# A looped part that is never entered, a lookup table handed over in two parts, and one transfer for q, k and the decay logits

## What is computed

```python
f = 1.0 / (1.0 + np.exp(-f_logit))
for t in range(S):
    state = f[:, :, t, :, None] * state + np.einsum('bhd,bhe->bhde', k[:, :, t], v[:, :, t])
    y[:, :, t] = np.einsum('bhd,bhde->bhe', q[:, :, t], state)
x = attn_out.transpose(0, 2, 1, 3).reshape(B * S, H * D)

logits = x @ w_gate + modality_bias[modality_id]
e_idx = np.argmax(logits, axis=1)
probs = np.exp(logits - logits.max(-1, keepdims=True)); probs /= probs.sum(-1, keepdims=True) + 1e-09
h = np.maximum(x[mask] @ w1[e], 0.0)
out[mask] = gate_w[mask, None] * (h @ w2[e])          # for each expert e

g = xn @ w_gate                                        # xn: x after RMS norm
return ((g * (1.0 / (1.0 + np.exp(-g)))) * (xn @ w_val)) @ w_out
```

## Time and profile before

| | us |
|---|---|
| median of 3 executions | 838.8 (836.85 to 844.91) |
| the profiled execution, its own time | 838.23 |
| its span, first to last instruction | 836.5 |
| TensorE busy in the span | 811.1 (97%) |
| DVE, ACT, GpSimd busy | 452.0, 380.0, 140.5 |

### The profile page before, as it was taken

How to read it: one execution, slowest core, us unless ns; L and a number is a source line. 1 busy time by engine, 2 the same in 40 slices (tenths; PEclk the granted TensorE clock), 3 DMA queues, 4 the chain that set the end, 5 groups by cost and what they waited for, 6 DMA issues and landing times.

```text
span 836.5 us, 15683 instructions
## 1 busy us (share of the span) xinstructions
PE 811.1 (97%) x5624; PEld 737.0 (88%) x5624; DVE 452.0 (54%) x715; ACT 380.0 (45%) x742; POOL 140.5 (17%) x170
## 2 busy tenths in 40 slices
PE   7999987799999999989999999999999999999997
PEld 6888877799999999988888888888988888888886
DVE  8989996886666666634433433333333334333331
ACT  6999975666665555534223312412332233122222
POOL 4003043785540000000001000200110010001001
PEclk9999998999999999999999999999999999999999
DMA  9979866998887977602002000200100000001000
GB/s 202 198 154 225 174 210 229 339 348 292 255 260 253 355 233 260 174 20 96 1 0 76 1 1 1 75 0 0 51 25 0 0 38 0 0 0 38 0 0 38
DMA packets 44121, 96.59 MB, mean 115 GB/s; under 512 B 9200, under 2 KB 25072, under 8 KB 43952
## 3 DMA queue, kind: packets, MB, share of 16 engines
q1 hardware_dynamic: 39984, 85.81, 34.7%
q0 software_dynamic: 3840, 9.47, 3.2%
q10 hardware_dynamic: 256, 0.79, 0.4%
HBM read 76.75 MB, written 19.29 MB: 115 GB/s over the span
## 4 chain that ended last, share of the span: by engine, by line
PE 88%; DVE 4%; issue 2%; ACT 2%; DMA 1%; POOL 0%; SPq 0%; DVEq 0%; ACTq 0%
PE h_ps L1887 16%; PE h_ps L1888 16%; PE h_ps L1886 16%; PE ym_ps L1886 7%; PE ym_ps L1888 7%; PE ym_ps L1887 7%; PE xTm_ps L1886 3%; PE xTm_ps L1888 3%; PE xTm_ps L1887 3%; PE sc_ps L839 2%; PE x_ps L859 2%; PE yT_ps L811 2%; PE ds_ps L783 1%; PE yT_ps L804 1%; PE turn_ps L830 1%
## 5 line engine op out<-in xcount | busy, mean ns | idle before, releaser
L1862 DVE TENSOR_TENSOR gs<-h_ps,sig 128x512 f32<-128x512 f32 x72 | 49.8, 692 | 177.2 <-ACT sig L1679 177.2
L1679 ACT ACTIVATE sig<-h_ps 128x512 f32<-128x512 f32 x72 | 43.1, 598 | 160.3 <-PE h_ps L1888 160.3
L1690 ACT CAST h_hi<-hid 128x512 fp32r<-128x512 f32 x72 | 44.6, 620 | 149.5 <-DVE hid L1865 149.5
L1886 PE MATMUL h_ps<-x_hi,w_hi 128*128 128x256 f32 x312 | 90.0, 289 | 8.4 <-DVE w_lo L271 4.5
L1887 PE MATMUL h_ps<-x_hi,w_lo 128*128 128x256 f32 x312 | 89.6, 287 | 0.0
L1888 PE MATMUL h_ps<-x_lo,w_hi 128*128 128x256 f32 x312 | 89.6, 287 | 0.0
L1888 PE MATMUL h_ps<-w_lo,wg_hi 128*128 128x512 f32 x216 | 85.2, 395 | 0.0
L1887 PE MATMUL h_ps<-w_hi,wg_lo 128*128 128x512 f32 x216 | 85.1, 394 | 0.0
L1886 PE MATMUL h_ps<-w_hi,wg_hi 128*128 128x512 f32 x216 | 84.1, 389 | 0.0
L1888 PE MATMUL h_ps<-w_lo,wv_hi 128*128 128x512 f32 x216 | 84.1, 389 | 0.0
L1886 PE MATMUL h_ps<-w_hi,wv_hi 128*128 128x512 f32 x216 | 84.0, 389 | 0.0
(11 more groups left out here) (237 smaller groups left out, 1790.3 us busy)
## 6 DMA issues: line engine op xcount, KB each, us to landing
w_raw<-in_w SPq DMA_DIRECT2D x52, 384.0 KB, 5.3
w_in<-in_w SPq DMA_DIRECT2D x52, 384.0 KB, 5.5
qkf_in<-in_qkf SPq DMA_DIRECT2D x43, 288.0 KB, 5.0
y_sorted<-x_tiles SPq DMA_DIRECT2D x13, 384.0 KB, 3.6
v_in<-in_v SPq DMA_DIRECT2D x24, 192.0 KB, 5.3
x_regions<-zero_row SPq DMA_DIRECT2D x12, 384.0 KB, 3.1
x_tiles<-x_regions SPq DMA_DIRECT2D x12, 384.0 KB, 4.0
g_in<-in_wg SPq DMA_DIRECT2D x3, 768.0 KB, 6.9
```

The lines of the kernel that those rows point to most:

```text
L1679: nc.scalar.activation(sig[:], g_ps, ACT.Sigmoid).then_inc(sig_done, 1)
L1690: nc.scalar.copy(h2_hi[:, fb % HELD], hid[:]).then_inc(h2_hi_done, 1)
L1862: nc.vector.tensor_tensor(gs[:], g_ps, sig[:], ALU.mult).then_inc(gs_done, 1)
L1886: nc.tensor.matmul(out, hi, rhs_hi, start=first, stop=False)
```

## The change

1. q, k and f of a tile lie in memory as 112 rows of 6144 bytes, with the 16 neutral rows among them, and one DMA of 112 partitions replaces two of 48 (`FIRST_LOADS` gives the new counts to wait for). The very first loads keep their form.
2. GpSimd no longer waits at the end of attention for its own scatters to land. `least` and `small`, from which the flag comes, are made one pipeline step earlier, and the flag's product stands ahead of `read` on TensorE.
3. In `general_attention` TensorE's part over tiles is a true loop of one body instead of code written out for four tiles and again for the last group. It reads its rows from a buffer `rows_in` of its own.
4. The table is made in two parts. Expert numbers and region ends are written straight to `table` (`table_ready` 1); rows, offsets and the count of tiles follow after `shifted_scores` (`table_ready` 2). SyncE loads w1 part 0 of tile 1 after the first, ahead of `pad`, and x and the later parts after the second.
5. In the first tile `place` stands ahead of `lo_w2(0, 0)`, the tiles of the experts behind lo_h(0), and `rows_of_tiles` and `gates_of_tokens` at the end of the tile instead of inside it. TensorE counts after hidden(0) instead of inside it.
6. ACT spreads its four `hi_w2(0, g)` over the tile, without a wait for SyncE's mark, and does one third of the dense weights (`hi_third(1)`) at the end. In all tiles the parts 2 and 3 of w2 are split at the start of the tile that uses them, not at the end of the one before. GpSimd's thirds wait for `w2_split` at 6 instead of `x_split` at 2.

The core of the diff:

```diff
             def load_qkf(c, b, n):
                 wait_past(sp, scaled, n - 3)
-                for par in range(2):
-                    sp.dma_start(qkf_in[par * PAD:par * PAD + D, b].rearrange("p a j t -> p (a j t)"),
-                                 qkf[n, par]).then_inc(qkf_landed[b], 16)
+                sp.dma_start(qkf_in[0:ROWS, b].rearrange("p a j t -> p (a j t)"), qkf[n]).then_inc(qkf_landed[b], 16)
...
-            for b in range(B):
-                pool.wait_ge(scattered[b], 16 * (LATE // B))
-            pool.wait_ge(scattered_late, 16 * B)
-            pool.wait_ge(ended, 16 * B)
...
-                def group(c):
-                    for b in range(B):
+                with pe.Fori(0, CH) as c:
+                    with pe.Fori(0, B) as b:
...
                 if place == "first":
                     sp.wait_ge(table_ready, 1)
                     e1 = expert(1)
-                    pad(e1)
                     for g in range(GR):
+                        sp.wait_ge(w1_split, g + 1)
+                        load_w1(e1, g)
+                        if g == 0:
+                            pad(e1)
                         if g == 1:
+                            sp.wait_ge(table_ready, 2)
                             sp.wait_ge(scattered, 16 * B)
                             load_x(1)
-                        sp.wait_ge(w1_split, g + 1)
-                        load_w1(e1, g)
...
-            pool.wait_ge(x_split, 2)
+            pool.wait_ge(w2_split, GR + 2)
...
-            lo_w2(0, 0)
             dve.wait_ge(counted, 1)
             rt.place(nc, dve, CH - 1, B, (CH - 1) * B, pre_ps, cnt_ps, marks, 0)
+            lo_w2(0, 0)
...
+                lo_h(0)
                 if place == "first":
                     tiles_of_experts()
-                lo_h(0)
-                if place == "first":
-                    table_of_tiles()
                 else:
+                    lo_w2(j, 2)
                     next_w1(0)
                 lo_h(1)
                 if place == "first":
                     lo_w2(0, 1)
                     shifted_scores()
-                    lo_w2(0, 2)
+                    table_of_tiles()
+                else:
+                    lo_w2(j, 3)
```

More of the change, by code:

```diff
@@ L438, in first_load @@
                 eng.wait_ge(pads_set[b], 1)
[L439 removed]
+                eng.dma_start(qkf_in[rows, b, 2].rearrange("p j t -> p (j t)"), qkf[b, rows, f_cols:]).then_inc(f_landed[b], 16)
             else:
@@ L846, in step @@
                     nc.tensor.matmul(flag_ps, rt.ones_r[:], small[:], start=True, stop=True).then_inc(flag_sum, 1)
+                    read(c, b, tile(c, b, 2))
                     pe.wait_ge(ks_done, GROWN)
@@ L1144, in group @@
                         mm.then_inc(lgt_done, 1)
-                    if not is_last(c):
+                    with pe.If(c < CH - 1):
                         pe.wait_ge(redone, c * Routing.PLACED + Routing.CHOSEN)
                         rt.count(nc, B, group_ps[:, 0], group_ps[:, 1]).then_inc(recounted, 1)
-                groups(pe, group)
                 first.turn(nc, pe, xT_ps, ident, again)
@@ L1607, in scalar @@
             act.wait_ge(shared.ahead.w2_landed, 16 * GR)
-            for g in range(GR):
-                hi_w2(0, g)
+            hi_w2(0, 0)
             def body(j, place):
@@ L1621, in next_w2, with own_w2 @@
                     if place != "last":
-                        act.wait_ge(y_part, j * PARTS + (g + 1 if g < GR - 1 else PARTS))
+                        act.wait_ge(y_part, j * PARTS + g + 1)
                         hi_w2(j + 1, g)
+                def own_w2(g):
+                    if place != "first":
+                        act.wait_ge(y_part, j * PARTS)
+                    hi_w2(j, g)
                 if place == "last":
@@ L1628, in body @@
                 hi_h(0)
-                if place != "first":
+                if place == "first":
+                    hi_w2(0, 1)
+                else:
+                    own_w2(2)
                     next_w1(0)
@@ L1632, in body @@
                 if place == "first":
-                    for i in range(EARLY):
-                        hi_third(i)
+                    own_w2(2)
+                    own_w2(3)
+                    hi_third(0)
                 else:
+                    own_w2(3)
                     next_w1(1)
@@ L1665, in body @@
                     nc.scalar.copy(y_kept_rows[:, s], y_ps[:, s, 0:DM]).then_inc(y_kept, 1)
-                next_w2(3)
+                if place == "first":
+                    next_w2(1)
+                    hi_third(1)
                 if place == "middle":
@@ L1830, in body @@
                 if place == "first":
+                    lo_w2(0, 2)
                     lo_w2(0, 3)
-                    rows_of_tiles()
                     next_w1(0)
@@ L1849, in body @@
                     next_w2(0)
+                    rows_of_tiles()
+                    gates_of_tokens()
                     next_w2(1)
-                next_w2(2)
-                next_w2(3)
             tiles(dve, body)
@@ L1911, in hidden @@
                     for i in range(2):
-                        if place == "first" and g == 0 and i == 1:
-                            pe.wait_ge(marks, Routing.CHOSEN)
-                            rt.count(nc, B, pre_ps, cnt_ps).then_inc(counted, 1)
                         cols = slice(i * P, (i + 1) * P)
@@ L1934, in body @@
                 hidden(0)
+                if place == "first":
+                    pe.wait_ge(marks, Routing.CHOSEN)
+                    rt.count(nc, B, pre_ps, cnt_ps).then_inc(counted, 1)
                 hidden(1)
```

59 lines of the change are left out of this document (32 added, 27 removed).

## The result

The changed kernel takes 851.88 us (median of 6 executions, 849.22 to 858.88) against 840.19 for the kernel before (6 executions): 1.0152 times as long, 95% interval 1.0095 to 1.0209. I had said 833, with a range that ended at 839.5. All ratios here leave out executions more than 1.5% above the fastest of their kernel, four in all: one of e7 (2801.15 us), one of e15 and two of the kernel before beside e9 to e11.

A forecast was written before the change was run, and what follows sets the result against it. TensorE, busy for 97% of 836.5 us, was taken to bound the kernel. From 838.23, -3.9 at tile 1's start and -1.5 + 0.3 in it (-5.1) gave 833.1, said as 833; range 829.5 to 839.5.

The forecast's parts named there:

- the sum: Whole kernel: -3.9 us at tile 1's start and -1.5 + 0.3 in it make -5.1.
- behind 177 us all moves up as a whole: Tiles after 177 us: TensorE has no holes there, so the earlier gain was to carry through unchanged.
- The jump: At attention's end: shorter skipped code starts TensorE 4.3 us earlier, and at full clock, which saves some 2.2 us.
- the sign that the prediction names: At attention's end: first h_ps product within 0.5 us of it, and a granted clock of 1.00 from 131 to 141.
- Loads for tile 1: First tile: earlier loads of w1 and x start tile 1 at 154.2 instead of 158.08, 3.9 us won.
- Tile 1: In tile 1: of the 2.70 us wait for h_lo, 1.5 won and 1.2 stay; 0.3 given back.
- so they fit: Past 165 us: three GpSimd operations in a row cost DVE 2.0 us, within h_lo's slack of 3.0.
- Attention: Steady attention: the 98 KB more that a tile moves stay hidden, so no time is won or lost.
- The rivals: Four outcomes: jump costs 4.5 us (0.27), loads sooner (0.08), GpSimd's thirds on h_lo (0.06), DMA-bound attention (0.04).
- Rival 3: Tiles 1 and 2: GpSimd's later thirds delay h_lo; two groups give +5.6 us, 838.7 or 843; chance 0.06.

The follow-up runs named there:

- e7: The kernel before with only one DMA of 112 partitions for q, k and f instead of two of 48; ratio 0.9998 to the kernel before.
- e15: e1 with SyncE's loads of the thirds behind the loads for the next tile; ratio 1.0062 to the kernel before.
- e9: e3 with GpSimd's subtractions and scatters mixed instead of three subtractions in a row; ratio 1.0003 to the kernel before.
- e11: The kernel before with only GpSimd's subtractions and scatters mixed; ratio 0.9975 to the kernel before.
- e2: The kernel before with only the split of w2's parts 2 and 3 moved into the tile that uses them; ratio 1.0157 to the kernel before.
- e5: The kernel before once more, unchanged, for a second profile; no time or ratio is given.
- e1: The changed kernel with w2's parts 2 and 3 split at the end of the tile before; 845.59 us against 846.69 for the kernel before, ratio 0.9999.
- e3: The changed kernel, late split kept, with SyncE's load of x ahead of the loads of w2's parts 2 and 3; ratio 0.9992 to the kernel before.
- e6: The changed kernel once more, unchanged, timed in turns with the kernel before on one chip; ratio 1.0137.
- e8: e1 with two DMAs of 48 partitions for q, k and f; ratio 1.0001 to the kernel before.
- e12: e3 with `rows_of_tiles` and `gates_of_tokens` back inside the first tile; 833.68 us against 839.1 for the kernel before, ratio 0.9936.
- e4: The kernel before with only TensorE's skipped part made a loop; ratio 1.000 to the kernel before.
- e13: e1 with `rows_of_tiles` and `gates_of_tokens` back inside the first tile; ratio 0.9989 to the kernel before.

## Why the prediction was wrong, point by point

- **The step that failed** is one that the sum does not have. Part 6 of the change splits parts 2 and 3 of w2 in the tile that uses them, in all tiles. I followed it through DVE's order in tile 1 only, and wrote that "behind 177 us all moves up as a whole, since TensorE has no holes there". The absence of holes says nothing of the slack. x was asked for 8.6 us ahead of its use, and some 4 of these are landing. The late split took all of the rest (x is asked for 3.9 to 4.0 us ahead in the later tiles, without a wait), and where GpSimd's thirds lengthen DVE's splits it took more, 2.6 us in the tile shown. I did not ask which of SyncE's loads wait for a split that moves, and what stands behind them. Price: 1.0157 by e2 alone, some 13 us; by the twelfth turn_x 8.5 to 11.4 us more than before in the two profiles of the changed kernel.
- **The jump (-4.3 us at the start, and -2.2 for the clock; in the sum only by way of the loads).** Its reading as a cost of the skipped code's length fell with e5, e2, e7 and e11. I took one execution for a property of the kernel. The block from q8 is no proof either: the same trace has one more between 115 and 121 us and one between 136 and 141, where TensorE is busy throughout. So the sign that the prediction names, no hole in the changed kernel, came true by luck. By the rule of the Trainium skill ("Runtime: NRT & Kernel Launch", section "Instruction fetch mechanics") a jump out of the window of two blocks must wait for a fetch. The traces bear that out neither way: the same code waits 4.46 us once and not at all in four other executions.
- **Loads for tile 1 (start at 154.2, -3.9).** Right in size: 22.8 us behind attention's end against 26.9, -4.1 (22.4 to 22.8 in e1, e3, e6, e8). But the working has two errors that cancel: w1 part 2 was issued 16.0 us behind attention's end (150.34), not 14.9, and landed in 3.9 us (ACT takes it at 154.28), not 5.3. Not all of the 4.1 is the new order's, either. With the old order and no hole tile 1 starts at 24.1 (e2) to 26.3 (e7). The rest, 1.3 to 3.9 us, is left to the earlier table with the loads behind it, which no run tried alone.
- **Tile 1 (-1.2).** 2.38 us of wait for h_lo stayed in the changed kernel, and 0.6 in e6, against 1.2 said. I had taken w1 part 3 as landed when the tile starts; it starts at 157.12, ACT gets that part only at 157.64, and DVE stands idle for 1.53 us. The waits for x ahead of the first two turn_x, 1.26 and 1.43 us, have no place in the sum; the wait for x_lo was 0.82, where 2 to 3 were said. That GpSimd's later start was harmless ("so they fit") was wrong. I priced its hold on DVE and forgot SyncE, which waits for GpSimd's thirds ahead of tile 3's weights. e12 shows what it cost on top of e3, 5.2 us.
- **Attention (0).** Right within the 0.3% of e7 and e8.
- **The rivals.** None was what happened. Rival 3 had the sign and the right culprit in part: GpSimd's thirds do come later and do hold DVE (4.42 us for one split). But it priced the hold by the slack of h_lo; what it made late was x, through SyncE's queue.
- **What e12 says of the sum.** -6.4 us at the twelfth turn_x, 0.9936 in time, that is -5.4 of 839.1. That this is near the -5.1 that I predicted, once the two things behind SyncE's waits are out of the way, is in part luck: e12 is at -6.1 by the second turn_x already, with the wait for h_lo in tile 1 down to under half a us, and with `rows_of_tiles` in another place than I had priced.
- **A slip.** 833.1 with the 0.6 that the text itself adds for the median is 833.7, not 833.

## What to carry to other kernels

When a step is moved later, list every semaphore that it feeds. For each queue that waits for one of them, look at what is issued next, not at what is waited for: here the split fed a w2 load that had time, and the x load behind it had none. A busy share of 100% shows no slack; take it from the trace as issue to use, less landing. And read two executions before an idle stretch whose named releaser can't be the true one enters a sum.

## What the runs showed of the hardware

Attention's end varies by up to 14 us between executions of nearly the same code (131.15 us in the earlier trace rows, 145.43 in e4), and by 11.7 us for the same kernel: 142.81 in e5. In e5 TensorE waits 1.55 us without a named releaser ahead of 111.34, and 1.75 for ACT ahead of 124.62. The granted clock is low behind each of them, and comes back to 1.00 between (length, busy us, clock, DMA share, GB/s):

```profile
111.00:115.00 4.00, 3.52 (x32) 3.11 (x36) 1.55 (x7) 3.97 (x12) 1.92 (x2) 0.52 0.55 164
119.00:123.00 4.00, 3.88 (x56) 3.21 (x56) 3.93 (x7) 3.00 (x9) 2.81 (x3) 1.00 0.66 249
125.00:129.00 4.00, 4.00 (x39) 3.43 (x38) 1.88 (x4) 1.29 (x5) 0.00 (x0) 0.50 0.45 142
```

The level at 0.50 is the lower one (1.2 GHz), and TensorE is busy throughout the last of these stretches. The kernel before had, in the execution of the earlier trace rows, a mean clock of 1.00 from 109 to 125 us, with waits of at most 1.02 us:

```profile
109.00:125.00 16.00, 13.79 (x204) 11.61 (x208) 15.36 (x42) 11.16 (x32) 6.85 (x7) 1.00 0.63 216
```

That mean is 1.00 in the two profiles that were compared first and in e13, 0.98 in e12, and between 0.61 and 0.89 in the rest, whatever the kernel. A wait of over a microsecond is not needed for it. In e12 the clock falls to 0.50 as well, though TensorE's last wait ahead of it is 0.68 us (at 122.29); the kernel before has the same wait at 122.63 and stays at 1.00 until attention's end:

```profile
125.00:129.00 4.00, 4.00 (x48) 2.89 (x42) 1.22 (x3) 1.55 (x4) 3.09 (x4) 0.50 0.87 259
```

What starts the fall was not tried, and stays open. It makes single executions differ by more than most of the edits do, which is why the second reading of each kernel here goes from attention's end.
